# Scoring the second router during the last expert of the first layer

## The chip, the cores and the metric

The program runs on one core of a Trainium2 chip. Its engines are named as in the profile: PE is TensorE (matrix products and, against an identity, transposes), PEld its weight load, ACT is ScalarE, DVE is VectorE, POOL is GpSimd, SP is SyncE, which here only issues transfers. The metric is the time of one execution on the device, in microseconds (us); lower is better.

## The reference

Three blocks follow each other on 1536 tokens of 512 numbers, in fp32. Block 1 is an attention with a window and four sink positions. Blocks 2 and 3 are mixtures of 8 experts (two matrices of 512 x 1024 and 1024 x 512 each). What matters here is the end of block 2 and the start of block 3:

```python
# block 2, in _moe_ref: two experts for each token
for e in range(E):
    for k in range(2):
        mask = top2[:, k] == e
        h = np.maximum(x[mask] @ w1[e], 0.0)
        out[mask] += top2_w[mask, k, None] * (h @ w2[e])
# block 3, in _moe2_ref, on x = out of block 2: one expert for each token
logits = x @ w_gate + modality_bias[modality_id]
e_idx = np.argmax(logits, axis=1)
gate_w = softmax(logits)[np.arange(N), e_idx]
```

Block 3's choice needs the complete sum over all experts of block 2, but its scores are linear in that sum.

## The kernel before

**First layer (block 2).** Each expert e owns 416 places ("slots"), in four groups of rows (k = 0 to 3; three of 128 and one of 32). `first1(e, f)` makes one of 8 pieces of the hidden layer, transposed, with 12 products of 416 columns. `second1(e, d)` makes one of 4 pieces of the expert's output with 24. Numbers are split into a high and a low part (fp32r), and so three products stand for one: ACT copies the high part out of PSUM (`relu1`, `x1_high_part`), DVE computes the low part (`h1_low_part`, `x1_low_part`). ACT copies each finished piece into `yT` (`y1_copy`). `back(e, k)` transposes `yT` into rows of tokens, `y_scale(e, k)` multiplies them by the gate on DVE into one of two row buffers, and `scatter1(e, k)` on POOL adds the rows to `x_moe1` in HBM with an indirect transfer. This way back of expert e-1 is interleaved with `first1(e, f)`, at f = 0, 2, 4, 6. `y_scale` waits until the scatter two places earlier has landed, since it writes the same buffer.

**Overflow.** Tokens that find no slot are treated by `over_layer`, which reads a count at run time and branches over its whole body when that is zero; with these inputs it is zero. PE, ACT, DVE and POOL each have such a branch, and SP one too. Before the change those of PE, ACT, DVE and POOL stand after expert 7.

**Between the layers.** When all scatters have landed, POOL raises `all_scattered`. SP then loads the 12 tiles of 128 tokens back (`x2_loads`, into `x2_rows`), PE transposes them (L1121), ACT and DVE split them (L1554, L2147), `group_scores` (L1104) multiplies by the second router's weights in three groups of four tiles, `turned_scores` (L1112) turns the scores to rows of tokens, and DVE adds the bias (`biased_scores`, L2143). `keep_clock_up(30)` (L770) is filler on PE for the time in which it waits for the tiles.

**Routing (after that).** `pick` (from L1765) finds each token's expert, `place_tokens(1)` its place, POOL writes one table (`coded_tiles`, L551) and DVE another (L1842), PE multiplies them (`codes2`, L881), and POOL gathers the rows of the first tile (L646). SP loads the first expert's weights once `order` is known. The second layer then runs over tiles.

Each engine runs its own program in order and is held only by semaphores, so the order in the code is that of the work.

## Time and profile before

| | us |
|---|---|
| three runs, median | 691.99 (690.84 to 693.63) |
| profiled execution, its own time | 693.64 |
| span of the profiled execution | 691.90 |
| PE busy, all of the span | 647.2 |
| expert 7, from its first product to its last | 414.91 to 452.91 |
| from there to the start of `pick` | 452.91 to 488.64 |
| first product of the second layer | 505.64 |

The span is what the trace covers. The execution's own time is 1.74 us more than it. Starts in the trace are counted from the span's start.

### The profile page before, as it was taken

How to read it: one execution, taken by the hardware profiler on the slowest of the kernel's cores; microseconds unless marked ns; L12 is line 12 of the kernel's file. 1: busy time of each engine (PE TensorE's matmuls, PEld its weight loads, DVE VectorE, ACT ScalarE, POOL GpSimd, SP SyncE). 2: the span in 40 equal slices, each digit the busy share in tenths (PEclk: the TensorE clock that was granted, in tenths of full speed). 3: DMA queues.
4: the chain of work that ended last, by engine and by line, in shares of the span. 5: the costliest groups of instructions: out<-in, count | busy, mean ns of one | idle time of the engine just before them, and what ended most of it. 6: DMA issues, size and time to landing. Idle time of an engine off the chain costs nothing. (4 is left out here: it accounts for less than half of the span.)

```text
span 691.9 us, 11241 instructions
## 1 busy us (share of the span) xinstructions
PE 647.2 (94%) x3822; PEld 581.3 (84%) x3823; DVE 317.1 (46%) x642; ACT 273.5 (40%) x525; POOL 183.1 (26%) x194
## 2 busy tenths in 40 slices
PE   8989999998999999999999999967489999999994
PEld 6989998897999999999999999944268888788883
DVE  4566646585456436262543624114684422452221
ACT  5768766333434244352524333104155321441210
POOL 2500100137172615425161512030131221221201
PEclk9999999999999999999999999999799999999998
DMA  7777630454584645556564502035396410001100
GB/s 212 266 271 259 222 118 23 169 170 133 172 245 153 146 139 113 180 153 185 152 155 123 108 3 34 12 47 182 122 358 221 157 56 31 30 24 42 46 15 26
DMA packets 52095, 91.21 MB, mean 132 GB/s; under 512 B 8591, under 2 KB 14735, under 8 KB 52048
## 3 DMA queue, kind: packets, MB, share of 16 engines
q1 hardware_dynamic: 41872, 69.21, 29.8%
q0 software_dynamic: 10176, 21.38, 13.9%
q8 instruction: 29, 0.48, 0.3%
q14 instruction: 18, 0.15, 0.1%
HBM read 74.52 MB, written 18.40 MB: 134 GB/s over the span
## 5 line engine op out<-in xcount | busy, mean ns | idle before, releaser
L588 POOL DMA_INDIRECT x_moe<-rows,dst_idx x29 | 57.8, 1994 | 138.0 <-DVE rows L1977 135.9
L1588 DVE TENSOR_TENSOR split<-stage,split 128x2048 fp32r<-128x2048 f32 x32 | 73.3, 2290 | 41.8 <-ACT split L1255 41.7
L900 PE MATMUL banks<-xTs,split 128*128 128x416 f32 (+1 forms) x256 | 88.6, 350 | 0.8 <-issue 0.8
L901 PE MATMUL banks<-xTs,split 128*128 128x416 f32 (+1 forms) x256 | 86.4, 342 | 0.0
L958 PE MATMUL banks<-hTs,split 128*128 128x416 f32 x224 | 79.6, 355 | 0.0
L959 PE MATMUL banks<-hTs,split 128*128 128x416 f32 x224 | 78.5, 351 | 0.0
L1390 ACT ACTIVATE hTs<-banks 128x416 fp32r<-128x416 f32 x56 | 29.0, 518 | 82.6 <-PE banks L903 82.6
L1255 ACT ACTIVATE split<-stage 128x2048 fp32r<-128x2048 f32 x32 | 60.9, 1908 | 0.5 <-DMA stage<-w1a 0.5
L1477 ACT ACTIVATE hTs<-banks 128x512 fp32r<-128x512 f32 x28 | 16.6, 597 | 108.0 <-PE banks L1178 108.0
L903 PE MATMUL banks<-xTs,split 128*128 128x416 f32 (+1 forms) x256 | 56.2, 340 | 0.0
L705 PE MATMUL banks<-k_sb,q_sb 128*128 128x260 f32 (+2 forms) x192 | 49.9, 386 | 2.9 <-DMA k_sb<-k_w 1.5
L1598 DVE CUSTOM_DVE_ANT_0 negs<-banks,masks 128x260 f32<-128x260 f32 (+2 forms) x96 | 35.0, 402 | 35.9 <-PE banks L705 34.6
L1750 DVE SCALAR_TENSOR_TENSOR hTs<-banks,hTs 128x416 fp32r<-128x416 f32 x56 | 32.8, 587 | 36.3 <-ACT hTs L1390 36.2
L900 PEld LDWEIGHTS banks<-xTs,split 128*128 128x128 f32 x256 | 48.1, 188 | 1.3 <-issue 1.0
L662 POOL DMA_INDIRECT out<-rows,dst x14 | 14.3, 1020 | 131.5 <-DVE rows L2070 131.5
L1268 ACT ACTIVATE probs<-negs,negmax 128x260 f32<-128x260 f32 (+2 forms) x96 | 46.1, 484 | 7.3 <-DVE negmax L1598 7.1
L901 PEld LDWEIGHTS banks<-xTs,split 128*128 128x128 f32 x256 | 48.2, 188 | 0.3
L1950 DVE TENSOR_TENSOR xTs<-banks,xTs 128x512 fp32r<-128x512 f32 (+1 forms) x28 | 16.6, 592 | 68.0 <-ACT xTs L1359 45.0
L965 PE MATMUL banks<-hTs,split 128*128 128x416 f32 x224 | 47.7, 355 | 0.0
L1163 PE MATMUL banks<-split,xTs 128*128 x112 | 45.3, 405 | 2.3 <-DVE split L1584 1.6
L903 PEld LDWEIGHTS banks<-xTs,split 128*128 128x128 f32 x256 | 46.2, 187 | 0.3
L1189 PE MATMUL banks<-split,hTs 128*128 x112 | 45.0, 402 | 0.6 <-ACT hTs L1477 0.6
(292 smaller groups left out, 1290.2 us busy)
## 6 DMA issues: line engine op xcount, KB each, us to landing
stage<-w1a SPq DMA_DIRECT2D x16, 1024.0 KB
stage<-w2a SPq DMA_DIRECT2D x16, 1024.0 KB, 5.5
k_sb<-k_w SPq DMA_DIRECT2D x12, 520.0 KB, 4.5
raw<-w1b SPq DMA_DIRECT2D x6, 1024.0 KB
raw<-w2b SPq DMA_DIRECT2D x6, 1024.0 KB, 7.0
q_sb<-q_t SPq DMA_DIRECT2D x24, 128.0 KB, 3.5
x_attention<-rows SPq DMA_DIRECT2D x12, 256.0 KB, 5.5
split<-x_moe SPq DMA_DIRECT2D x12, 256.0 KB, 5.2
```

Of the source, the lines that this page charges most:

```text
L588: pool.indirect_dma_start(out=x_dram[1], out_offset=rows_at(dst_idx[0], early_dst, e, k), in_=y_room(n), in_offset=None, compute_op=ALU.ad ...
L705: mm = pe.matmul(S[:, j % 2, h, 0:n], q_sb[:, b, pair, h, :], k_sb[:, b, pair, 0:n], start=True, stop=True)
L900: pe.matmul(psum, piece(slot, 0, o + c * FH), xTs[:, 0, c, 0:cols], start=(c == 0), stop=False)
L901: pe.matmul(psum, piece(slot, 1, o + c * FH), xTs[:, 0, c, 0:cols], start=False, stop=False)
L903: mm = pe.matmul(psum, piece(slot, 0, o + c * FH), xTs[:, 1, c, 0:cols], start=False, stop=(c == DC - 1))
L958: pe.matmul(psum, piece(e % 2, 0, o), hTs[:, 0, c, 0:cols], start=(c == 0), stop=False)
L959: pe.matmul(psum, piece(e % 2, 1, o), hTs[:, 0, c, 0:cols], start=False, stop=False)
L965: mm = pe.matmul(psum, piece(e % 2, 0, DC * F + c * D + d * P), hTs[:, 1, c, 0:cols], start=False, stop=(c == FC - 1))
L1163: pe.matmul(psH[:, half, :], xTs2[:, 0, c, :], weights(slot, 0, o), start=(c == 0), stop=False)
L1255: act.activation(split_chunk(e % 2, 0, c), staged_chunk(e % 2, c), ACT.Copy).then_inc(high_done[c], 1)
L1268: act.activation(probs[:, b, 2 * pair + h, 0:span(kind)], negs[:, j % 2, h, 0:span(kind)], ACT.Exp, bias=negmax[:, j % 2, h:h + 1], scale= ...
L1588: dve.tensor_tensor(split_chunk(e % 2, 1, c), staged_chunk(e % 2, c), split_chunk(e % 2, 0, c).bitcast(F32), ALU.subtract).then_inc(low_do ...
```

## The change

The second router's scores are computed in two parts. The rows that lack only expert 7's share are loaded, transposed and scored while PE works on expert 7. Expert 7's share comes another way: `last_logits(d)` multiplies its unscaled outputs in `yT` by the router's weights in fp32, giving 8 scores for each slot; DVE multiplies these by the gate and cuts them in three bf16 parts (`last_tokens`); `last_to_tokens` adds them to their tokens with 48 products against one-hot tables that DVE makes of the slots' tokens (`last_away`, `last_one_hot`); DVE sums everything. What goes with it:

- `most_scattered` is raised when the scatters up to expert 6 have landed, and `x2_loads` waits for that. Its buffer is now a ring of 8 tiles in expert 6's weight room; tiles 8 to 11 wait for a transpose each.
- The way back of expert 6 stands at f = 0, 1, 2, 3 of expert 7.
- All `over_layer` parts now stand between expert 6 and expert 7 (on POOL ahead of expert 6's scatters).
- Expert 7's rows are turned into four banks and scaled by ACT (`last_scale`), no longer by DVE. Its scatters stay ahead of `coded_tiles(1)` on POOL.
- `keep_clock_up(30)` goes.

```diff
-        x2_rows = split[:, 1, 0].bitcast(F32)[:, 0:TILES * D].rearrange("p (t d) -> p t d", d=D)
+        x2_ring = split[:, 0, :, DC * TILES * P:].bitcast(F32).rearrange("p k (t d) -> p k t d", d=D)
@@ SP
-            sp.wait_ge(all_scattered, 1)
+            sp.wait_ge(most_scattered, 1)
             for t in range(TILES):
+                if t >= 8:
+                    sp.wait_ge(x2t, t - 7)
+                sp.dma_start(x2_row(t), x_dram[1][t * P:(t + 1) * P, :]).then_inc(x2_in[t % 8], 16)
@@ POOL
             for e in range(1, E):
+                if e == E - 1:
+                    over_layer()
                 for k in range(SUBS if e > 1 else EARLY_SUBS + 1):
                     scatter1(e - 1, k)
+                if e == E - 1:
+                    all_landed(nth_sub(e, 0))
+                    pool.sem_inc(most_scattered, 1)
@@ PE, new functions
+            def x2_transposes(t):
+                pe.wait_ge(x2_in[t % 8], 16 * (t // 8 + 1))
+                if t >= 4:
+                    pe.wait_ge(x2t_low, t - 3)
+                for c in range(DC):
+                    mm = pe.transpose(ps2T[:, t % 4, c * P:(c + 1) * P], x2_row(t)[:, c * P:(c + 1) * P], ident[:])
+                mm.then_inc(x2t, 1)
+            def last_logits(d):
+                pe.wait_ge(y1_copied, DC * (E - 1) + d + 1)
+                if d == 0:
+                    pe.wait_ge(scaled1, nth_sub(E - 1, 0))
+                for k in range(SUBS):
+                    first = min(k * P, SLOTS - P)
+                    mm = pe.matmul(psLast[:, k, :], yT[:, d, first:first + P], wg2[:, d, :], start=(d == 0 and k == 0),
+                                   stop=(d == DC - 1 and k == SUBS - 1), skip_group_check=True)
+            def last_to_tokens():
+                pe.wait_ge(last_hots, SUBS)
+                pe.wait_ge(last_parted, 1)
+                for t in range(TILES):
+                    for k in range(SUBS):
+                        mm = pe.matmul(psMore[:, t, :], last_hot[:, k, t, :], last_parts[:, k].rearrange("p n e -> p (n e)"),
+                                       start=(t == 0 and k == 0), stop=(t == TILES - 1 and k == SUBS - 1), skip_group_check=True)
+                mm.then_inc(last_added, 1)
@@ PE, the experts
+                    elif e == E - 1 and f < SUBS:
+                        pe.wait_ge(scaled1, nth_sub(e - 1, f))
+                        back(e - 1, f, psO1)
...
+                if e == E - 2:
+                    over_layer()
+            last = E - 1
+            second1(last, 0)
+            for t in range(3):
+                x2_transposes(t)
+            second1(last, 1)
+            last_logits(0)
+            for t in range(3, 7):
+                x2_transposes(t)
+            second1(last, 2, groups=(0,))
+            last_logits(1)
+            for t in range(7, TILES):
+                x2_transposes(t)
+            second1(last, 3, groups=(1, 2))
+            last_logits(2)
+            turned_scores()
+            last_logits(3)
             for k in range(SUBS):
-                pe.wait_ge(scaled1, nth_sub(E - 1, k) - (k > 0))
-                back(E - 1, k, (psO1, psX1)[k % 2])
+                back(last, k, banks[:, k + 1, :])
+            last_to_tokens()
-            keep_clock_up(REST_LAYER, psH1[:, 0, :])
@@ ACT, expert 7 (x2_high is the copy that stood in L1554, turned_copy that of L1550)
+                y1_copy(last, 0)
+                for t in range(3):
+                    x2_high(t)
+                y1_copy(last, 1)
...
+                y1_copy(last, 3)
+                for k in range(SUBS):
+                    last_scale(k)
@@ DVE, after expert 7's low parts (x2_low is the operation of L2147)
+                last_away()
+                for t in range(TILES):
+                    x2_low(t)
+                    if t % 3 == 2:
+                        last_one_hot(t // 3)
+            def last_tokens():
+                dve.wait_ge(last_lg_ready, 1)
...
+                link(dve.tensor_tensor(last_parts[:, :, 2, :], last_rest, last_parts[:, :, 1, :], ALU.subtract))
+                dve.sem_inc(last_parted, 1)
+                dve.wait_ge(lg2, 1)
+                link(dve.tensor_tensor(noisy[:], ps2, bias_tok[:], ALU.add))
+                dve.wait_ge(last_added, 1)
+                link(dve.tensor_reduce(rb[:], psMore.rearrange("p t (n e) -> p t e n", e=E), AX.X, ALU.add))
+                link(dve.tensor_tensor(noisy[:], noisy[:], rb[:], ALU.add))
```

On PE's program, the place between expert 6's last products (L965 before, L992 now) and expert 7's first (L900 and L901 before, L925 and L926 now). Before:

```order
L965 MATMUL banks<-hTs,split 128x416 x8
L900 MATMUL banks<-xTs,split 128x416
L901 MATMUL banks<-xTs,split 128x416
```

Of the change, first the branch and then, behind the body that it jumps over, the end of the body and the products that follow:

```order
L992 MATMUL banks<-hTs,split 128x416 x8
L1095 TENSOR_LOAD used
L1095 ISA x2
L1096 COMPARE_AND_BRANCH
...
L1096 UNCONDITIONAL_BRANCH
L925 MATMUL banks<-xTs,split 128x416
L926 MATMUL banks<-xTs,split 128x416
```

The load of the count and the branch over the overflow's body now stand between two products that followed each other directly.

On PE's program, from expert 7's last products to the first product of the routing (L860 before, L885 now). Before:

```order
L965 MATMUL banks<-hTs,split 128x416 x8
L1018 MATMUL banks<-ident,yT 128x128 x16
L1069 TENSOR_LOAD used
L1069 ISA x2
L1070 COMPARE_AND_BRANCH
...
L770 MATMUL banks<-ones_bf 128x512 x30
L1121 MATMUL banks<-ident,split 128x128 x24
L1104 MATMUL banks<-split,wg_parts 16x512 x8
L1121 MATMUL banks<-ident,split 128x128 x16
L1104 MATMUL banks<-split,wg_parts 16x512 x8
...
L860 MATMUL banks<-chosen,ones_bf 128x8 x12
```

And of the change:

```order
L992 MATMUL banks<-hTs,split 128x416 x8
L1027 MATMUL banks<-wg,yT 128x8 x4
L1018 MATMUL banks<-both,rows 128x8 x12
L1027 MATMUL banks<-wg,yT 128x8 x4
L1091 MATMUL banks<-ident,yT 128x128 x16
L1037 MATMUL banks<-chosen,last_hot 128x24 x48
L885 MATMUL banks<-chosen,ones_bf 128x8 x12
```

The transposes of the token tiles and their scores are gone from this stretch; four sets of fp32 products come, two of them here (L1027), and the 48 one-hot products (L1037; the parts are kept in `chosen`).

On POOL's program, from the overflow's count to the first table of the routing, with the semaphores that each waits for. Before, expert 6's and expert 7's scatters, the count, the table:

```order
L588 DMA x_moe<-rows,dst_idx 1664x512 [waits scaled1,scattered1_1,scattered1_0]
L588 DMA x_moe<-rows,dst_idx 1664x512 [waits scaled1] x3
L621 TENSOR_LOAD used [waits fresh_ready0,scattered1_1,scattered1_0]
...
L551 TENSOR_TENSOR moving<-xT,code 128x12x19 [waits hot_ready]
```

And of the change:

```order
L613 TENSOR_LOAD used [waits fresh_ready0]
...
L603 DMA x_moe<-rows,dst_idx 1664x512 [waits scaled1,scattered1_1,scattered1_0]
L603 DMA x_moe<-rows,dst_idx 1664x512 [waits scaled1] x3
L603 DMA x_moe<-rows,dst_idx 1664x512 [waits scattered1_0,scattered1_1,scaled1]
L603 DMA x_moe<-rows,dst_idx 1664x512 [waits scaled1] x3
L567 TENSOR_TENSOR moving<-xT,code 128x12x19 [waits scattered1_0,scattered1_1,hot_ready]
```

The count moved ahead of both experts' scatters; the table still waits until expert 7's scatters have landed.

## Rows read from the trace of the kernel before

**Rows 1.** The page, busy time of each engine over the span.

```profile
PE 647.2 (94%) x3822; PEld 581.3 (84%) x3823; DVE 317.1 (46%) x642; ACT 273.5 (40%) x525; POOL 183.1 (26%) x194
```

**Rows 2.** Busy time by stretch: length, engines, granted clock (1.00 is full), DMA share, GB/s.

```profile
414.91:452.91 38.00, 38.00 (x209) 37.20 (x208) 9.80 (x14) 7.94 (x13) 6.33 (x4) 1.00 0.16 21
452.91:488.64 35.73, 25.80 (x142) 14.96 (x142) 11.31 (x19) 8.72 (x16) 6.27 (x4) 0.95 0.43 111
488.64:505.64 17.00, 7.06 (x58) 3.52 (x59) 13.41 (x45) 5.08 (x5) 3.71 (x7) 0.70 0.55 182
461.00:463.00 2.00, 2.00 (x6) 0.64 (x5) 0.00 (x0) 0.00 (x0) 1.69 (x2) 0.50 1.02 138
463.00:465.00 2.00, 2.00 (x9) 0.85 (x8) 0.00 (x0) 0.00 (x0) 0.15 (x1) 0.81 0.62 92
```

**Rows 3.** The chain that ended last, in order of time: start, length, what.

```profile
461.59 4.65 DMA x_moe<-rows,dst_idx
...
467.60 0.34 SPq L361
...
486.50 1.89 PE banks L1112 x16
...
488.64 0.27 DVE top L1765
```

**Rows 4.** The timeline of PE: start, length, what, count, idle before.

```profile
451.24 1.67 PE L965 MATMUL banks<-hTs,split 128*128 128x416 f32 x8
455.08 1.32 PE L1018 MATMUL banks<-ident,yT 128*128 128x128 f32 x8 [0.41 <-DVE rows L1977]
460.85 8.06 PE L770 MATMUL banks<-ones_bf 128*128 128x512 bf16 x30 [4.46 <-issue]
470.35 0.66 PE L1121 MATMUL banks<-ident,split 128*128 128x128 f32 x4 [1.44 <-DMA split<-x_moe]
477.41 1.91 PE L1121 MATMUL banks<-ident,split 128*128 128x128 f32 x16
480.02 2.01 PE L1104 MATMUL banks<-split,wg_parts 128*16 128x512 f32 x8 [0.70 <-DVE split L2147]
```

**Rows 5.** Two branches on PE's queue, by line: durations in ns, starts.

```profile
L1070 PEldq COMPARE_BRANCH  x1: 4037/4037/4037, 456.8 to 456.8; - x1
L1233 PEldq COMPARE_BRANCH  x5: 77/208/208, 623.4 to 673.6; - x5
```

**Rows 6.** Queue of instruction transfers (packets, MB, share), in 416:417 and in 458:459.

```profile
q8 instruction: 1, 0.02, 8.2%
q8 instruction: 1, 0.02, 5.9%
```

**Rows 7.** The timeline, small products on PE and a sum on DVE.

```profile
59.80 1.02 PE L764 MATMUL banks<-wg,xT 128*128 128x16 f32 x8
498.00 0.56 PE L881 MATMUL banks<-moving,row_hot 128*128 128x38 bf16 x12 [6.77 <-DVEq L1849]
498.74 0.31 DVE L1783 TENSOR_REDUCE owner_f<-shared 128x19 f32<-128x152 f32 x1
```

**Rows 8.** The timeline, expert 7: ACT behind `first1(7, 1)` and `(7, 2)`, POOL's first scatter.

```profile
420.04 0.52 ACT L1390 ACTIVATE hTs<-banks 128x416 fp32r<-128x416 f32 x1 [2.17 <-PE banks L903]
422.29 0.52 ACT L1390 ACTIVATE hTs<-banks 128x416 fp32r<-128x416 f32 x1 [1.74 <-PE banks L903]
424.98 0.52 ACT L1390 ACTIVATE hTs<-banks 128x416 fp32r<-128x416 f32 x1 [2.17 <-PE banks L903]
421.80 1.62 POOL L588 DMA_INDIRECT x_moe<-rows,dst_idx  x1 [20.21 <-DVE rows L1977]
```

**Rows 9.** The timeline, the two tables of the second routing.

```profile
495.71 0.57 POOL L551 TENSOR_TENSOR moving<-xT,code 128x228 bf16<-128x228 f32 x1 [32.56 <-DVEq L1839]
495.71 2.18 DVE L1842 TENSOR_TENSOR row_hot<-row_i,iota_row 128x1536 bf16<-128x1536 int32 x1
```

**Rows 10.** Transfers to and from `x_moe`, issue to landing.

```profile
DMA to landing us min/median/max: 2.7/4.9/12.2
```

More of the change, by code:

```diff
@@ L584, in scatter1 @@
                 if k == 0 and e > 0:
[L585 to L586 removed]
+                    all_landed(n)
                 pool.wait_ge(scaled1, n + 1)
@@ L944, in early_second_low, with second1 @@
                 mm.then_inc(y1, 1)
-            def second1(e, d, between=None):
+            def second1(e, d, between=None, groups=()):
                 cols = SLOTS
@@ L961, in second1 @@
                     x1_transposes(e + 1, between)
+                for g in groups:
+                    group_scores(g)
                 for c in range(FC):
@@ L966, in second1, with group_scores @@
                 mm.then_inc(y1, 1)
+            def x2_transposes(t):
[5 more added lines that the diff above has]
+                mm.then_inc(x2t, 1)
+            def group_scores(g):
+                pe.wait_ge(x2t_low, (g + 1) * GROUP)
+                if g == 1:
+                    pe.wait_ge(lg2t_copied, g)
+                for c in range(DC):
+                    for k in range(2):
+                        mm = pe.matmul(ps2L[g], wg2_parts[:, c].rearrange("p k e -> p (k e)"),
+                                       x2T[:, k, c, g * GROUP:(g + 1) * GROUP, :].rearrange("p t n -> p (t n)"),
+                                       start=(c == 0 and k == 0), stop=(c == DC - 1 and k == 1))
+                mm.then_inc(lg2t, 1)
@@ L1055, in _ @@
                             back(0, k, psO1)
-                    elif f % 2 == 0:
+                    elif e < E - 1 and f % 2 == 0:
                         pe.wait_ge(scaled1, nth_sub(e - 1, f // 2))
                         back(e - 1, f // 2, psO1)
-                for d in range(DC):
-                    more = e < E - 1
-                    second1(e, d, {1: 1, 2: 3}.get(d) if more else None)
-                    if more and d < 2:
-                        x1_transposes(e + 1, 2 * d)
-            for k in range(SUBS):
-                pe.wait_ge(scaled1, nth_sub(E - 1, k) - (k > 0))
-                back(E - 1, k, (psO1, psX1)[k % 2])
@@ new lines, in first_layer @@
+                    if more:
+                        for d in range(DC):
+                            if d in (1, 2):
+                                x1_high_part(e + 1, 2 * d - 1)
+                            y1_copy(e, d)
+                            if d < 2:
+                                x1_high_part(e + 1, 2 * d)
+                            else:
+                                first_layer_high(e + 1, d)
+                    if e == E - 2:
+                        over_layer()
+                last = E - 1
@@ new lines, in first_layer @@
+                y1_copy(last, 0)
+                for t in range(3):
+                    x2_high(t)
+                y1_copy(last, 1)
+                for t in range(3, 7):
+                    x2_high(t)
+                turned_copy(0)
+                y1_copy(last, 2)
+                for t in range(7, TILES):
+                    x2_high(t)
+                turned_copy(1)
+                turned_copy(2)
+                y1_copy(last, 3)
+                for k in range(SUBS):
+                    last_scale(k)
```

327 lines of the change are left out of this document (168 added, 159 removed).

## The prediction

> **What bounds the kernel now.** I first read the page's engine shares: PE is busy 94% of the span and all others are below half [rows 1], so a change is worth what it takes off PE's idle or wasted time, or off a chain on which PE waits. Then the busy times by stretch. In expert 7 PE is busy 38.00 of 38.00 us at full clock, with DVE, ACT and the transfers nearly free. In the 35.73 us between expert 7's last product and `pick` it is busy 25.80, and 8.06 of these are the 30 filler products [rows 2, 4]. The routing behind that is a chain on DVE, 17.00 us long, which the change leaves as it is [rows 2]. Third, the chain that ended last, between 453 and 489: the last scatter lands at 461.59 + 4.65 = 466.24, SP issues the loads from 467.60, PE starts on the tiles at 470.35, and the last turned scores end at 488.39 [rows 3, 4]. So this stretch waits on a round trip through HBM, and then on PE, ACT and DVE in turn; the filler costs nothing there. The change puts the round trip and the tiles' work under expert 7, where PE has no idle time: what PE does in there lengthens it in full.
>
> **The change part by part.** I count PE's time from 452.91, the end of expert 7's last product, to `pick`; 35.73 us before. A product that follows its like is priced by the start-to-start time of its row.
>
> What stays or comes, on PE, all of it uncovered:
> - Twelve tiles of four transposes: 16 took 1.91 us, so 0.48 for a tile, 5.7 us [rows 4].
> - Three groups of scores of 8 products: 2.01 us each, 6.0 us [rows 4].
> - Twelve turned scores: 16 took 1.89 us, so 1.4 us [rows 3].
> - Sixteen fp32 products of `last_logits` with 8 columns. No row has these; the nearest is the first router's, fp32 with 128 x 128 weights and 16 columns, 8 in 1.02 us, so 2.0 us. The 0.118 us of a turned score as a lower end gives 1.9.
> - Four ways back: a `first1` with one takes 424.98 - 422.29 = 2.69 us and one without 422.29 - 420.04 = 2.25, so 0.44 each, 1.8 us [rows 8].
> - 48 one-hot products in bf16, 24 columns. The nearest is `codes2`, bf16, 38 columns, 12 in 0.56 us, so 2.2 us; at the price of the fp32 row it would be 6.1, the upper end [rows 7]. I take the bf16 row.
> - DVE's end: a sum over 288 numbers (0.31 us for 152 [rows 7], so some 0.45), an addition like the 0.27 us steps of `pick` [rows 3], and about 0.2 for two semaphores: 0.95 us. DVE's five small steps on the slots' scores, some 1.3 us, lie under the four ways back (1.8); without that cover they would cost 1.3.
>
> Together 20.05 us.
>
> What is moved: the overflow's branch. On PE the gap around it is 456.40 to 460.85, 4.45 us, 4.04 of it the branch instruction itself [rows 4, 5]. Before, that lay in the time in which PE waited for the tiles anyway. Now it stands between two products that followed each other without a gap, and nothing hides it: +4.45. Other branches of PE take 0.08 to 0.21 us [rows 5]. They jump over one tile's step; this one jumps over about 200 matrix products with their weight loads. A transfer of instructions stands in the microsecond from 458 on, inside the long branch [rows 6]: I read it as the code behind the body being fetched. The body is as long as before. In the undisturbed stream a transfer also stands in 416:417, some 1.5 us behind the branch's new place [rows 6], so the code there is near the end of what was brought in, and the target is again beyond what follows. The Trainium skill, "Advanced Engine Details and Errata" (Control Flow Timing), gives about 108 ns for a compare-and-branch. By that price the gap would be about 0.5 us and the sum 4 us smaller. The Trainium skill, "Runtime: NRT & Kernel Launch" (Instruction fetch mechanics), says that a taken branch whose target is outside the fetched window stalls until it is brought in. By that the 4.45 comes again; the trace agrees with it, with 4.04 us against 0.21.
>
> The clock: after the gap at 456.40 the granted clock is 0.50 in 461 to 463 and 0.81 in 463 to 465 [rows 2], that is at 1.2 GHz until about 463.76, or 2.9 us after work resumed, half of which is lost: +1.45 us for the same gap ahead of expert 7. Ahead of it PE is busier than it was ahead of 456.40, so the fall may not come; the bounds are 0 and 1.45, and I take 1.45, as the only gap of this length had it.
>
> ACT, DVE and POOL have their own branches in the same place. They wait for PE there and have short bodies; I cost them at nothing, and DVE's low parts have until four `first1` later.
>
> Waits that come in. `y_scale(6, 2)` needs the first scatter's buffer. That scatter started at 421.80 [rows 8] and landed 4.65 us on [rows 3], at 426.45, and its scale takes some 0.7. PE, with a way back behind each `first1`, wants that scale for `back(6, 3)` at 424.98 + 0.44 = 425.4 [rows 8], so it would wait 1.8 us. But the gap on PE gives DVE time to catch up, so that the first scatter can start closer behind PE; then nothing is left of the wait. I take 0.3 and keep 0 and 1.8 for the range. Behind the waiting scale on DVE stands the low part of f = 3, needed only by `first1(7, 7)`. With the shift of 5.9 us and the late start kept, the first scatter starts at 427.7, the second 2.69 later at 430.4, and lands at 435.05; the fourth waits for that and starts some 1.6 later, landing at 441.3. SP issues the loads 0.4 on, and the first tile is there 2.75 us after its issue (470.35 against 467.60 [rows 3, 4]), near 444.5. PE wants it after `second1(7, 0)`: 414.91 [rows 2] plus 8 x 2.25, 4 x 0.44, 4.56 for the 24 products (a quarter of what is left of the 38.00) and 6.2 of gap, clock and wait, so 445.4. Hidden, with 0.9 us to spare. The last tiles wait a little on DVE's pace: 0.2. Together +0.5.
>
> On POOL the first table waits for expert 7's scatters. The first scale starts about 4.6 us ahead of `pick`, the fourth scatter is issued near 2.6 us after it and lands near 7.3. The table was made 495.71 - 488.64 = 7.07 after `pick` and takes 0.57, and PE needs it only with DVE's table, which ends 2.18 us after it starts [rows 9]. So 7.9 against 9.3: hidden by 1.4 us. The gather is later still, and so the whole rest moves with `pick`.
>
> The sum: 20.05 + 4.45 + 1.45 + 0.5 = 26.45 us against 35.73, that is -9.3 us. The profiled execution's span of 691.90 becomes 682.6 and its time of 693.64 becomes 684.3. The median of the runs lies 1.65 below that execution, so I forecast 691.99 - 9.3 = 682.7. A measurement of this kernel can tell about 0.5%, or 3.5 us, from no change.
>
> **The rivals.**
>
> (a) *The forecast*, 682.7, with 681 to 687 for the open prices: the clock that may not fall (-1.45), the wait of `back(6, 3)` (up to +1.5), one-hot products at up to 6.1 (+3.9, of which I allow 3). Chance 0.63.
>
> (b) *The moved branch is cheap.* If the target's code is at hand in the new place, the branch costs the 0.21 us of PE's others, and the clock doesn't fall: 682.7 - 3.8 - 1.45 = 677.4. For it: all other branches. Against it: the same body, and rows 6. By the 108 ns of the Trainium skill, "Advanced Engine Details and Errata" (Control Flow Timing), this would be the case. Chance 0.15.
>
> (c) *POOL becomes the bound after `pick`.* If a scatter of expert 7 takes not 4.65 us but the longest landing of `x_moe`, 12.2 us [rows 10], the table is 7.5 later, less the 1.4 spare: 682.7 + 6.1 = 688.8, the same as before or just faster. The long landing may be one of the large transfers to `x_moe`, and in this stretch little else moves until the weights' loads. Chance 0.09, with all cases in which half or more of the gain is lost to some wait.
>
> (d) *Slower: the scatters of expert 6 hold PE.* They go in two rounds, each waiting for the one before. Each us that a landing takes beyond 4.65 brings the tiles 2 us later, less the 0.9 spare, and PE stands in expert 7 waiting for the first tile. At 12.2 us: 2 x 7.55 - 0.9 = 14.2, so 696.9. The gain is gone from a landing of about 9.8 us on, and the kernel slower by 0.5% from 11.5. Against it: the transfers are busy 0.16 in expert 7 [rows 2], and 4.65 was measured with four scatters in a row. Chance 0.06.
>
> (e) *The change does little*, since the fp32 products or the table of expert 7 take several times their nearest rows: 687 to 690. Chance 0.07.
>
> **How the numbers follow.** The likeliest is (a), 682.7. From 676.5, below (b), to 688, short of (c), lie (a), (b) and about half of (e): 0.8. Faster by over 0.5% is below 688.5: (a), (b), and half of (c) and (e), 0.86. Within 0.5%: 0.08. Slower: (d), 0.06.
>
> **What the profile after would show.** A gap of about 4.4 us on PE between L992 and L925 and a long branch at L1096, with a granted clock of 0.5 for some 3 us behind it (right for (a)); none of the two (b). PE without a wait for tiles at L1000 (d would show it there, and on DVE a long wait ahead of the scale of group 2). Expert 7, gap aside, about 15 us longer. From the end of the last L992 product to `pick` some 7.5 us where it was 35.73. `L567` no later than about 8 us after `pick`'s start and L906 no later than 9.4 (c shows otherwise). I would be wrong above all if the one-hot products or `last_logits` are far from their rows, or the landing is slower with the new rhythm.

## The result, and the profile after

Times in us, each median over the runs of the same session on one chip, with the ratio of the changed kernel to the kernel before and its 95% interval:

| session | before | changed | ratio |
|---|---|---|---|
| first | 692.62 (690.84 to 693.63) | 684.15 (682.01 to 686.54) | 0.9881 [0.9832, 0.9931] |
| second | 692.0 | 683.17 (682.49 to 689.22) | 0.9892 [0.986, 0.9925] |
| third | 691.62 | 683.87 (681.05 to 686.87) | 0.989 [0.9864, 0.9917] |

The change saves 7.8 to 8.8 us, 1.1 to 1.2%. The profiled execution took 682.12 us, with a span of 680.2. It lies 2.0 below its median, where that of before lay 1.0 above the median in the table (1.65 above that of the three runs known ahead of the prediction), so the difference of the two spans, 11.7 us, is larger than what the change gives. What follows is therefore read by stretches. Most of the spread between runs lies ahead of the place that was changed: in the thirteen profiles of the changed kernel and its variants, whose code is the same up to there, expert 6's last product ends between 412.4 and 417.5, while from there to `pick` the three profiles of the changed kernel took 62.90, 62.73 and 62.91 us. What sets the time ahead of it is open.

The page of the changed kernel, busy time of each engine and the granted clock in 40 slices. PE has 50 more instructions and is busy 1.6 us less than in [rows 1]:

```profile
PE 645.6 (95%) x3872; PEld 585.2 (86%) x3873; DVE 322.6 (47%) x651; ACT 276.2 (41%) x529; POOL 185.5 (27%) x194
PEclk9999999999999999999999999998599999999997
```

Busy time by stretch of the changed kernel (columns as in [rows 2]): expert 7; from its last product to `pick`; from `pick` to the second layer's first product; and four pieces of the second stretch:

```profile
414.50:466.36 51.86, 51.03 (x299) 46.74 (x299) 24.19 (x33) 14.84 (x27) 6.33 (x4) 1.00 0.30 77
466.36:476.20 9.84, 8.96 (x105) 8.75 (x103) 1.91 (x8) 3.27 (x5) 2.70 (x2) 0.83 0.11 13
476.20:493.89 17.69, 8.37 (x58) 3.92 (x59) 13.58 (x45) 5.19 (x5) 9.26 (x10) 0.61 0.84 227
470.00:471.00 1.00, 1.00 (x10) 1.00 (x11) 0.05 (x1) 0.00 (x0) 0.00 (x0) 1.00 0.00 0
471.00:472.00 1.00, 1.00 (x8) 1.00 (x7) 0.86 (x5) 0.43 (x1) 0.00 (x0) 0.57 0.00 0
472.00:474.00 2.00, 2.00 (x13) 1.94 (x12) 0.28 (x2) 1.63 (x3) 0.81 (x1) 0.50 0.00 0
474.00:475.00 1.00, 1.00 (x43) 1.00 (x42) 0.00 (x0) 0.69 (x1) 0.77 (x1) 0.72 0.00 0
```

Against [rows 2], expert 7 is 13.86 us longer (51.86 for 38.00), the way to `pick` 25.89 shorter (9.84 for 35.73), and the routing 0.69 longer. The routing's end is a gather that landed after 3.91 us in this run. What follows it, to the end of the span, is 186.31 us long, and was 186.26. So the gain lies in the place that was predicted; of the 11.7 us between the spans 1.8 are none of it, since expert 6's last product already ended at 413.30 for 415.07. The last four lines show what was not: PE is busy without a break, and the granted clock falls from full to half at about 471.1.

The timeline of PE in the changed kernel (start, length, what, count, idle before), from expert 6's last products to the codes. L1091 is a way back, L1000 the tiles' transposes, L1009 the group scores, L1027 `last_logits`, L1018 the turned scores, L1037 the one-hot products, L906 `codes2`:

```profile
411.63 1.67 PE L992 MATMUL banks<-hTs,split 128*128 128x416 f32 x8
414.50 0.43 PE L925 MATMUL banks<-xTs,split 128*128 128x416 f32 x1 [1.21 <-issue]
...
425.70 0.66 PE L1091 MATMUL banks<-ident,yT 128*128 128x128 f32 x4 [0.63 <-DVE rows L2067]
...
439.77 1.47 PE L1000 MATMUL banks<-ident,split 128*128 128x128 f32 x12
...
464.69 1.67 PE L992 MATMUL banks<-hTs,split 128*128 128x416 f32 x8
466.20 0.95 PE L1027 MATMUL banks<-wg,yT 128*128 128x8 f32 x8
467.08 2.84 PE L1018 MATMUL banks<-both,rows 16*128 16x8 f32 x24
469.86 1.06 PE L1027 MATMUL banks<-wg,yT 128*128 128x8 f32 x8
470.77 3.32 PE L1091 MATMUL banks<-ident,yT 128*128 128x128 f32 x16
473.88 1.43 PE L1037 MATMUL banks<-chosen,last_hot 128*128 128x24 bf16 x48
...
485.83 0.56 PE L906 MATMUL banks<-moving,row_hot 128*128 128x38 bf16 x12 [6.57 <-DVEq L1940]
```

The reader is to see three things. PE stands idle 1.21 us where the branch is now, not 4.45. The first tile's transposes (L1000) wait for nothing. And the counts of L1027 and L1018 are twice those of the code: four fp32 products of `last_logits(d)` are 8 records, 12 turned scores are 24.

By line, the branch and the load of its count on PE's own queue in the changed kernel (durations in ns, starts); the like of before is in [rows 5]:

```profile
L1096 PEldq COMPARE_BRANCH  x1: 3712/3712/3712, 410.6 to 410.6; - x1
L1095 PEldq TENSOR_LOAD <-used x1: 488/488/488, 409.8 to 409.8; - x1
```

The branch is nearly as long as it was, 3.71 us for 4.04. But it starts at 410.6, while the last product of expert 6 ends at 411.63 + 1.67 = 413.30: PE's queue had come to it 2.7 us before the array had worked off the products ahead of it, and only what outlasts them is seen.

### The profile page after: what moved, and what is told of

It is laid out like the page before. It is cut to its first block, busy times and chain, and to the rows that moved or that the text cites. A ratio compares the mean times of both kernels' runs of the same rounds, so it can differ in the third digit from the quotient of the medians.

```text
span 680.2 us, 11358 instructions
## 1 busy us (share of the span) xinstructions
PE 645.6 (95%) x3872; PEld 585.2 (86%) x3873; DVE 322.6 (47%) x651; ACT 276.2 (41%) x529; POOL 185.5 (27%) x194
## 4 chain that ended last, share of the span: by engine, by line
PE 83%; DVE 6%; DMA 3%; ACT 2%; issue 2%; SPq 1%; ACTq 0%; POOL 0%; DVEq 0%; POOLq 0%
PE banks L984 6%; PE banks L983 6%; PE banks L992 6%; PE banks L925 5%; PE banks L926 5%; PE banks L928 5%; PE banks L730 5%; PE banks L758 4%; PE banks L1234 4%; PE banks L1239 4%; PE banks L1235 4%; PE banks L1260 4%; PE banks L1261 4%; PE banks L1264 3%; PE banks L742 2%
## 5 line engine op out<-in xcount | busy, mean ns | idle before, releaser
L925 PE MATMUL banks<-xTs,split 128*128 128x416 f32 (+1 forms) x256 | 88.9, 352 | 2.0 <-issue 2.0
L926 PE MATMUL banks<-xTs,split 128*128 128x416 f32 (+1 forms) x256 | 86.4, 342 | 0.0
L925 PEld LDWEIGHTS banks<-xTs,split 128*128 128x128 f32 x256 | 48.1, 188 | 2.9 <-issue 2.5
L926 PEld LDWEIGHTS banks<-xTs,split 128*128 128x128 f32 x256 | 48.2, 188 | 0.3
L992 PE MATMUL banks<-hTs,split 128*128 128x416 f32 x224 | 47.7, 355 | 0.0
L2191 DVE TENSOR_TENSOR hTs<-banks,hTs 128x512 fp32r<-128x512 f32 x28 | 19.2, 690 | 58.0 <-ACT hTs L1581 57.1
```

The lines of the kernel that those rows point to most:

```text
L925: pe.matmul(psum, piece(slot, 0, o + c * FH), xTs[:, 0, c, 0:cols], start=(c == 0), stop=False)
L926: pe.matmul(psum, piece(slot, 1, o + c * FH), xTs[:, 0, c, 0:cols], start=False, stop=False)
L992: mm = pe.matmul(psum, piece(e % 2, 0, DC * F + c * D + d * P), hTs[:, 1, c, 0:cols], start=False, stop=(c == FC - 1))
```

## The experiments

Each was run beside the kernel before on the same chip; a ratio is always to that. The first four were run in the second session of the table, the next four in one with a median before of 694.18 and without the changed kernel (so only their ratios are compared), the last four in the third of the table. "First product to `pick`" is the time from expert 7's first product to the start of `pick`, in the profiled execution. It is 61.70 us in the changed kernel, and was 73.73.

**The changed kernel again**, as the base of the next three experiments and for the spread.

> The changed kernel itself, for its spread: its four runs were 682.0, 682.1, 686.2 and 686.5 us, with mean granted clocks of 0.983, 0.982, 0.977 and 0.978. Theory: the 4 us between the two groups are one more stretch at half clock (0.0055 of 684 us is 3.8 us of full clock lost), so each run here falls in one of the two groups and its time follows its clock. Rival: the groups differ at equal clock, by transfers.

683.17, ratio 0.9892. First product to `pick` 61.92, the idle time at the branch 0.81, the wait of the fourth way back 1.22. So single profiles of one kernel differ by half a microsecond in these waits, while their sum stays (1.84 and 2.03, and 1.89 in the third profile below). The times fall in no two groups by their clock: three runs with a mean granted clock of 0.981 took 682.70, 683.48 and 685.76.

**Without PE's branch.** It leaves out PE's part of the overflow (with these inputs it has nothing to do).

```diff
             for e in range(1, E):
 ...
-                if e == E - 2:
-                    over_layer()
```

> Leaves out PE's part of the overflow layer, its branch included (unused with these inputs). Theory: the branch hides behind the products that PE has queued, and costs the 1.2 us that the trace after shows as a gap ahead of expert 7's first product, so 1.2 us are saved. Rival, as the prediction had it: the branch costs 4.45 us and 1.45 of clock, so up to 5.9 us are saved.

682.27, ratio 0.9858 [0.9834, 0.9882]: by the medians 0.9 us faster than the changed kernel beside it, and within its spread. The gap is gone, and two waits for DVE's scales stand in its place:

```profile
414.75 0.60 PE L1091 MATMUL banks<-ident,yT 128*128 128x128 f32 x4
418.56 0.66 PE L1091 MATMUL banks<-ident,yT 128*128 128x128 f32 x4 [0.96 <-DVE rows L2065]
421.34 0.60 PE L1091 MATMUL banks<-ident,yT 128*128 128x128 f32 x4
425.04 0.66 PE L1091 MATMUL banks<-ident,yT 128*128 128x128 f32 x4 [0.83 <-DVE rows L2065]
```

The pause at the branch had given DVE time, as the prediction supposed; without it PE waits 1.79 us for the scales, and 1.22 for one of them in the kernel above. From expert 6's last product to `pick` it is 62.80 us, for 62.73 to 62.91 with the branch: the 1.2 us expected are not saved there, let alone 5.9.

**The branch without its head start.** One wait holds PE's queue ahead of the branch until ACT has copied expert 6's last piece, so that nothing is queued behind which the branch could run.

```diff
                 if e == E - 2:
+                    pe.wait_ge(y1_copied, DC * (E - 1))
                     over_layer()
```

> PE waits until expert 6's last piece has been copied, and only then comes to the branch; nothing is queued behind which it could hide. Theory (the head start is what makes the branch cheap): the gap becomes some 5 us (0.7 for the copy, 0.7 for the count, 3.7 for the branch) against 1.2, +3.9 us, and the granted clock may fall behind it, +1.5 more; 688 to 690. Rival (the branch is cheap in its new place for another reason, such as code that is at hand): +0.7 us for the wait alone.

688.13, ratio 0.9949 [0.993, 0.9967]: 4.96 us slower than the changed kernel beside it, as the head start would have it. In its timeline and its windows:

```profile
412.41 1.67 PE L992 MATMUL banks<-hTs,split 128*128 128x416 f32 x8
419.42 0.69 PE L925 MATMUL banks<-xTs,split 128*128 128x416 f32 x1 [5.34 <-issue]
```

```profile
414.08:419.42 5.34, 0.01 (x1) 0.04 (x1) 2.45 (x2) 2.31 (x2) 0.00 (x0) 0.72 0.02 3
419.42:422.42 3.00, 3.00 (x9) 2.87 (x10) 0.00 (x0) 0.00 (x0) 0.00 (x0) 0.50 0.02 5
```

The same branch (3.69 us here) costs a gap of 5.34, and behind it 3 us at half clock, which are the two terms of the prediction (4.45 and 1.45) come true. What the prediction lacked is the head start, and this one edit takes it away. Some 0.6 us of the gap are the edit's own, since it also waits for ACT's copy (the load of the count starts at 414.7, the products end at 414.08).

**One-hot products between the ways back.** Expert 7's second pair of ways back goes behind `last_to_tokens`, so that DVE's end lies beside it.

```diff
-            for k in range(SUBS):
+            for k in range(2):
                 back(last, k, banks[:, k + 1, :])
             last_to_tokens()
+            for k in range(2, SUBS):
+                back(last, k, banks[:, k + 1, :])
```

> Two of expert 7's four ways back stand behind the 48 one-hot products instead of ahead of them. Theory (PE's order up to pick is the bound there): pick starts 1.6 us earlier after expert 7's last product, as two ways back took 1.6 us at half clock. On POOL the fourth scatter is issued no later, since POOL takes 1.87 us for each, but its landing now holds the first table: 1.2 to 1.6 us saved. Rival (POOL's wait for the scatters is already the bound): nothing saved, since the first table cannot come earlier than the landing.

684.01, ratio 0.9867 [0.9842, 0.9893], the same as the changed kernel; the 1.2 to 1.6 us expected do not show. `pick` comes no sooner in this run (first product to `pick` 62.39), since the clock fell 2.6 us behind expert 7's last product, in the turned scores already, ahead of the first thing that the edit moves. And the codes now wait for POOL, at the time at which they came anyway (9.79 us after `pick`, for 9.45 to 9.98 in the three profiles of the changed kernel):

```profile
PE banks L906 <- POOL moving L567: 7.1, 1, 7.1
```

The table came 8.32 us after `pick` (7.34 in the changed kernel), since the scatters ahead of it started later relative to `pick`. It cost nothing here; the account of POOL's table below says why.

**Turned scores earlier.** Two thirds of the turned scores go between the group scores and the last eight products of expert 7, to have fewer small products in a row behind it.

```diff
+                if len(groups) > 1:
+                    turned_scores((0, 1))
...
-            turned_scores()
+            turned_scores((2,))
```

> The turned scores of the first two groups stand inside expert 7's last piece, among its wide products, and only the third group's behind it. PE's work is the same. Theory (the granted clock falls in the tail because PE runs only small products for about 4.8 us there): with 2.9 us of them left ahead of the ways back, the clock stays at 1.00 until the ways back, which take 1.8 us and not 2.8 to 3.2, and from the last product of expert 7's piece to pick it is 9.8 - 1.85 - 1.2 = 6.7 us; the whole from expert 7's first product to pick is 1 to 1.5 us shorter. Rival (the clock falls at its own times): the whole is the same as before, 61.7 to 62 us.

686.03, ratio 0.9892 [0.9861, 0.9924]. The clock fell all the same, 3.4 us behind the last product, and the ways back took 2.98 us. So fewer small products in a row did not keep it up in this run. First product to `pick` is 63.12, longer than either theory had it, and 2.06 of it are a wait of the fourth way back of expert 6 for its scale, ahead of everything that the edit moves.

**Both of these.**

> The early turned scores together with two ways back behind the one-hot products. Theory: the tail is shorter by the 1.2 of the clock and by 0.9 for two ways back at full clock; but the first table waits for the fourth scatter's landing, which is 1.2 to 1.6 us later relative to pick, so part of it comes back as a wait of codes for POOL: 1 to 2 us below the changed kernel, 681 to 682. Rival (POOL holds it all): no more than the early turned scores alone.

685.17, ratio 0.9861 [0.9831, 0.989], not to be told from the changed kernel. First product to `pick` 61.62. In this run the clock stayed full until after the first pair of ways back (1.07 us for two, 1.95 for the two at half clock), and yet next to nothing was won up to `pick` (61.61 to 61.92 in the changed kernel); why is open. The codes waited for POOL's table again (6.6 us), but came 9.49 us after `pick`, no later than in the changed kernel.

**Expert 6's ways back at the old, even places.** This puts them behind `first1` 0, 2, 4, 6 as before, so that each scale finds its buffer free, but the scatters come later.

```diff
-                    elif e < E - 1 and f % 2 == 0:
+                    elif f % 2 == 0:
...
-                    elif e == E - 1 and f < SUBS:
-                        pe.wait_ge(scaled1, nth_sub(e - 1, f))
-                        back(e - 1, f, psO1)
```

> Expert 6's way back stands at f = 0, 2, 4, 6 of expert 7 again, everything else as changed. Theory: the wait of 0.6 to 1.2 us of PE for the third scale goes, but the fourth scatter is issued about 5.5 us later (434.5), lands at 439.2, and the first tile is there at 442.3 where PE wants it at 439.9 less the wait: 2 to 3 us of waiting for tiles appear, net 1 to 2 us slower. Rival (the landing has slack enough): 0.6 to 1.2 us faster.

689.36, ratio 0.9943 [0.9922, 0.9964]. First product to `pick` 67.03, which is 5.3 more, where 1 to 2 were expected. Counted from expert 7's first product (418.49 in this run, 414.50 in the changed kernel), the fourth scatter starts after 19.95 us for 14.10, SP's loads after 23.74 for 18.03, and PE waits for the first tile. The timeline of PE and two windows:

```profile
444.99 2.20 PE L1000 MATMUL banks<-ident,split 128*128 128x128 f32 x12 [1.93 <-DMA split<-x_moe]
```

```profile
446.00:448.00 2.00, 1.89 (x10) 1.62 (x9) 1.43 (x3) 1.48 (x3) 0.00 (x0) 0.69 0.90 306
448.00:450.00 2.00, 2.00 (x7) 1.89 (x7) 2.00 (x2) 0.00 (x0) 0.00 (x0) 0.50 1.03 370
```

A wait of 1.93 us is followed by some 3 us at half clock, which costs about 1.5 us more. That is rival (d)'s place, reached by a later start instead of a slower landing. It shows that a tile's wait would have been dear. Not all of the 5.3 us is the price of the rhythm, though: 1.9 lie behind expert 7's last product (11.76 us to `pick` for 9.84), where the clock fell 3.7 us behind it for 4.8.

**Filler among the turned scores.** Ten filler products of 512 columns, two behind every second score.

```diff
                 for t in range(TILES):
 ...
+                    if t < TILES - 1 and t % 2 == 1:
+                        keep_clock_up(2, banks[:, 1, :])
```

> Ten filler products of 512 columns (2.1 us) stand between the turned scores. Theory (it is the small products that let the clock fall): the granted clock stays 1.00 through the ways back, which then take 1.8 us and the one-hot products less too; from expert 7's end to pick 9.8 + 2.1 - 1.5, so about 10.5 us: 0.6 slower, with the clock up. Rival (the clock falls at its own times): the clock falls all the same, and the tail is 2.1 us or more longer.

689.9, ratio 0.9939 [0.99, 0.9978]. The clock fell at about 471.0, in the middle of the filler, and stayed low:

```profile
469.00:471.00 2.00, 2.00 (x12) 1.19 (x12) 0.00 (x0) 0.00 (x0) 0.00 (x0) 0.98 0.00 0
471.00:473.00 2.00, 2.00 (x7) 1.05 (x6) 0.00 (x0) 0.00 (x0) 0.00 (x0) 0.50 0.00 0
```

From expert 7's last product to `pick` it took 16.56 us for 9.84. The ten fillers themselves took 3.6 us, start to start, for the 2.1 expected, and the small products and ways back behind them more than before, at half clock. Filler on the critical path cost three times its price and bought nothing.

**The changed kernel a third time**, as the base of the last three.

> The changed kernel once more, as the base of the three others on this chip. Every theory expects a ratio to the kernel before of about 0.989 (0.986 to 0.993), expert 7's first product to pick 61.7 to 62.0 us.

683.87, ratio 0.989, first product to `pick` 61.61.

**Four rooms for expert 6's rows.** Groups 2 and 3 are scaled into `x_rows`, free at that time, and need not wait for the first scatters (POOL's scatters read them there).

```diff
...
+                own = e == E - 2 and k >= 2
-                if n >= 2:
+                if n >= 2 and not own:
...
-                dve.tensor_scalar(y_rows[:, n % 2], rows_in,
+                dve.tensor_scalar(x_rows[:, k - 2] if own else y_rows[:, n % 2], rows_in,
```

> Expert 6's third and fourth group of rows are scaled into a room of their own, so that DVE's scales of these groups no longer wait until the scatters of the first two have landed. Theory (the wait ahead of back(6, 3) is the only idle time of PE in expert 7 that the change brought): the idle time of 0.6 us (0.35 to 2.1 in the runs so far) ahead of the last way back of expert 6 is gone, the tiles' loads are issued earlier by 1 to 4 us, and the stretch from expert 7's first product to pick is 0.6 to 1.5 us shorter than in the changed kernel on this chip, ratio to the kernel before some 0.001 to 0.002 lower. Rival: the idle time is replaced by another (the way back waits on DVE's pace in any case, or the clock falls as much later), and the stretch stays within 0.3 us.

682.94, ratio 0.9867 [0.9841, 0.9893]. PE's waits of expert 7 in the changed kernel, and then in this one (line waited for: us in total, times, longest):

```profile
PE banks L925 <- issue: 1.2, 1, 1.2
PE banks L1091 <- DVE rows L2067: 0.6, 1, 0.6
PE banks L1000 <- DVE split L2109: 0.2, 1, 0.2
```

```profile
PE banks L927 <- issue: 0.8, 1, 0.8
PE banks L1002 <- DVE split L2112: 0.2, 1, 0.2
```

The wait is gone, and expert 7 takes 51.15 us for 51.85 in the changed kernel beside it. But in this run the clock fell 3.8 us behind the last product instead of 4.9, and the way to `pick` took 10.80 for 9.76. So expert 7's gain is shown in the trace; in the whole time, 0.9 us between medians is less than the spread.

**No share at all.**

```diff
-            last_logits(0)
...
-            last_to_tokens()
```

(and DVE's steps on them, and its sum).

> Leaves out expert 7's share of the scores altogether: no fp32 products of its slots, no one-hot products, none of DVE's steps on them, no sum; the second router then chooses from scores without that share, so places and tables can differ. It prices the way by which the share comes. Theory (all of it is uncovered on PE): 3.3 us of fp32 products, 1.24 of one-hot products, 0.75 of DVE's end go, so pick comes 5 to 6 us sooner behind expert 7's first product, and the kernel is 4 to 6 us faster than the changed one if POOL's table holds. Rival 1: pick no longer waits for the ways back, so it comes sooner still (by 3 more us, 8 to 9), but POOL's table, which waits for the scatters behind these ways back, then holds the codes' products; the gain up to the codes is then only 2 to 4 us. Rival 2: part of the share's way lies beside other work, and the gain is under 3 us throughout.

680.86 (680.70 to 681.19), ratio 0.9838 [0.9808, 0.9868], 3.0 us faster by the medians, though the two intervals just meet. First product to `pick` is 54.32, 7.3 us less; but the codes come 16.74 us after `pick` for 9.98, so that expert 7's first product to the codes is 71.06 for 71.59. The chain of this kernel, in order of time, shows what took over:

```profile
470.53 1.36 POOL x_moe L603
...
476.15 8.19 DMA x_moe<-rows,dst_idx
484.54 0.58 POOL moving L567
485.21 0.55 PE banks L906 x12
```

Rival 1 holds: of 7.3 us, 0.5 are left at the codes in this pair of profiles (and 1.2 at the second layer's first product, 77.84 for 79.04), less than the 2 to 4 that it named. The medians differ by its 3.0; the profile of the changed kernel beside it was the lowest of its six runs, so how much is left in the others is open. The last of its four scatters landed only after 8.19 us here, and the table waits for it. What came in its way can be read: with `pick` earlier, SP issued the second layer's first two weight loads of 1 MB each at 476.56, 0.41 us behind this scatter, and the transfers moved 316 GB/s from 480 to 484. In the three profiles of the changed kernel the loads came 2.8 to 3.7 us behind the last scatter. That they made it slow is likely, but no run held them back. The share's way on PE and DVE, and the scatters on POOL, run side by side and are nearly equal in length, so taking one away is worth little. That is rival (c), half a step away.

**Four rooms and the split together.**

> The four rooms together with expert 7's one-hot products moved between its second and third way back (their DVE end then lies beside two ways back). If both small gains hold and add, the ratio to the kernel before is about 0.985 to 0.987, that is 1.5 to 3 us faster than the changed kernel on this chip; from expert 7's last product to pick some 1.5 us less. Rival: POOL's table then comes as the last (8.3 us after pick or later, since the scatters start later relative to pick), and the gain of the split is lost to it: the ratio is that of the four rooms alone.

681.12 (680.07 to 685.26), ratio 0.9841 [0.9816, 0.9866]. The changed kernel beside it had 0.989 [0.9864, 0.9917]: five of its six runs lie below 683.0, and only one of the changed kernel's six does. The means are 681.9 and 684.0. The profiled run was its slowest, 685.26, and has the split's known end:

```profile
483.54 1.15 POOL L567 TENSOR_TENSOR moving<-xT,code 128x228 bf16<-128x228 f32 x1 [2.72 <-POOLq L663]
...
492.56 1.09 PE L1219 MATMUL banks<-ident,rows 128*128 128x128 f32 x4 [3.17 <-DMA rows<-x_moe,src]
```

First product to `pick` is 61.05, 0.6 less. The table starts 8.55 us after `pick`, the codes come after 9.79 as without the split, and the transposes ahead of the second layer's first product waited 3.17 us for their rows, for 0.71 and 1.60 in the first two profiles of the changed kernel. So by its median this is the best version of those that compute everything, 2.75 us below the changed kernel, and likely but not surely better; each half alone could not be told from the changed kernel.

## Why the prediction was right, and where its terms were not

The forecast was 682.7, 9.3 us below; measured were 7.8 to 8.8 below, with 684.15 well inside the range. Rival (a) holds as a picture: the round trip and the tiles' work are hidden under expert 7, `pick` comes close behind it, and the rest moves with `pick`. From the end of expert 6's last product to `pick`, the changed kernel took 476.20 - 413.30 = 62.90 us against 488.64 - 415.07 = 73.57: 10.7 us less in these two profiles, where the sum said 9.3. With 0.4 to 0.7 us lost in the routing, some 10 us are left at the second layer's first product, in all three profiles of the changed kernel; the medians say 7.8 to 8.8. There is one profile of before, and what the rest is stays open. The terms, in us:

| term | predicted | measured |
|---|---|---|
| branch | 4.45 | 1.2 (0.8 to 1.3 in three profiles) |
| clock behind it | 1.45 | 0 |
| twelve tiles | 5.7 | 5.3 |
| three group scores | 6.0 | 5.55 |
| `last_logits` | 2.0 | 3.4 |
| turned scores | 1.4 | 2.8 |
| ways back of expert 7 | 1.8 | 3.1 |
| one-hot products | 2.2 | 1.4 |
| DVE's end | 0.95 | 0.8 |
| waits in expert 7 | 0.5 | 0.8 |

These add to 24.35 us; the stretch itself is 25.06 (62.90 less the 37.84 from expert 6's end to expert 7's before), so 0.7 is not placed. The sum of the prediction was 26.45. The result is near the forecast because two groups of errors nearly cancel: 4.7 us too much for the branch and its clock, 4.1 too little for the small fp32 products and the ways back. The place of the gain was foreseen; that the total comes so near is luck.

**The moved branch (mis-sized, 4.45 + 1.45 against 1.2 + 0).** The step said that the branch "now stands between two products that followed each other without a gap, and nothing hides it". The products queued ahead of it hide it: its start, 410.6, is 2.7 us ahead of the end of expert 6's last product. The run that took the head start away had a gap of 5.34, half clock for 3 us behind it, and lost 4.96 us. In [rows 4, 5] it had no such cover. The last ways back, which end at 455.08 + 1.32 = 456.40, had waited for DVE's scale (0.41 us), so little was queued, and the branch started at 456.8, behind their end. So rival (b) was near with the size of the gap and wrong about its reason: the branch is not cheap, 3.3 to 3.8 us in four profiles of the new place, it is covered. Why it takes so long wasn't tried; that code is fetched, as [rows 6] was read, stays a reading. For it: in all five profiles read for this (before, the changed kernel three times, and the run without a head start) a transfer of instructions starts 0.6 to 1.7 us behind the branch's start, 411.5 to 412.0 in the changed kernel, and the run without PE's branch has none there. The price of the Trainium skill, "Advanced Engine Details and Errata" (Control Flow Timing), about 108 ns, fits neither place; by it, the gap of 5.34 could not be there. The Trainium skill, "Runtime: NRT & Kernel Launch" (Instruction fetch mechanics), describes a stall for a target that isn't at hand; the trace agrees in kind, with 3.3 to 4.0 us and the transfer inside them, but the page names no length.

**Small fp32 products (mis-sized).** `last_logits` is 0.80 to 0.91 us for four products, 0.21 each, and a turned score 0.23, where I took 0.125 and 0.118. The counts in the rows misled me: an fp32 product with moving columns leaves two records, so the row of the first router, x8 in 1.02 us [rows 7], is four products, and the x16 of [rows 3] eight turned scores, not sixteen. The code would have told: `x_logits` makes 4 products in each of 12 blocks, and the trace of before has 96 records of that line. Read so, the same rows give 16 x 0.255 = 4.1 us, an upper bound for half as many columns (3.4 measured), and 12 x 0.236 = 2.8 (2.8). The transposes leave one record each, which is why the ways back and tiles did not suffer from this.

**The ways back of expert 7 (mis-sized, by the clock).** Their 1.8 us became 3.1 since the granted clock was at half from 471.1, with PE busy in all of the time before. The prediction put the low clock behind the branch; it came behind the small products instead. In all thirteen profiles, of six different orders of this end, it fell between 2.6 and 5.4 us after expert 7's last product, and neither fewer small products nor ten wide fillers among them prevented it. Nine of the thirteen have the same work on PE from that product to the fall, and these nine alone span the whole range. So the order of the end is not what sets the moment, and one profile of an order cannot show that it moved it; what does set it is open.

**One-hot products** took 1.4 us, partly at half clock: 30 ns each, below the bf16 row. The upper end of 6.1 was far off.

**Waits.** The wait of the fourth way back is there, 0.6 us (0.59 to 1.22 in the three profiles of the changed kernel), within its bounds of 0 and 1.8; in the run with the turned scores earlier it was 2.06. The first tile had more to spare than predicted: issue at 432.53, wanted at 439.77, so some 4.5 us for 0.9. The forecast had kept the late start of before (421.80 [rows 8], 6.9 us behind expert 7's first product) and added 5.9 us of gap and clock. The first scatter started at 420.06, 5.6 us behind, and nearly all of the 5.9 was not there. SP's loads followed the fourth scatter's start by 3.93 us, too, where the forecast had 4.65 + 0.4. Rival (d) was therefore further off than it looked, and the run with even places shows what it would have cost.

Rival (e) had a grain of truth: the fp32 products cost 1.7 and 2 times what I took, which is 2.8 us, short of the 4 or more that it wanted.

**POOL's table** was done 7.91 us after `pick`, for 7.9 predicted (its start was at 7.34), and the codes waited for DVE (L1940), as said. But the forecast took the two tables as independent, and they are not. In the changed kernel's first and second profile:

```profile
483.54 2.18 DVE L1933 TENSOR_TENSOR row_hot<-row_i,iota_row 128x1536 bf16<-128x1536 int32 x1
483.54 0.57 POOL L567 TENSOR_TENSOR moving<-xT,code 128x228 bf16<-128x228 f32 x1 [3.16 <-DVEq L1930]
...
483.93 1.76 DVE L1933 TENSOR_TENSOR row_hot<-row_i,iota_row 128x1536 bf16<-128x1536 int32 x1
484.00 2.13 POOL L567 TENSOR_TENSOR moving<-xT,code 128x228 bf16<-128x228 f32 x1 [2.67 <-POOLq L661]
```

Started together, POOL's table takes 0.57 us and DVE's 2.18. Started 0.07 us later, POOL's takes 2.13 and ends 0.44 behind DVE's, which takes 1.76. In the two splits and in the run with both edits POOL's starts 0.36 to 1.05 later and again ends 0.43 or 0.44 behind. So they take turns (what makes them was not tried), and any lateness makes POOL's the last, in the changed kernel itself too. It costs nothing up to 1.05 us: the codes start 2.29 us behind DVE's table in all five of these profiles. Only without the share, where POOL's table started 6.5 us late, did it hold the codes.

## What to carry to other kernels

A branch, or any long instruction of an engine's queue, costs only what outlasts the work already queued ahead of it: look for its start in the queue's rows, and compare it with the end of that work, ahead of pricing a move. Where a stall is taken away, look for the next releaser of the same instruction within a microsecond: here the branch, DVE's scales and POOL's scatters each stood ready to take over, and removing one gave back little of its length (at the codes, 0.5 us of 7.3 in the profiles without the share). Where an engine is named as the one that was waited for, look also whether the work came later than before: POOL was named in four profiles in which nothing was lost. And ahead of pricing by a row's count, check what one record is against a loop whose count the code tells.

## What the runs showed of the hardware

- The granted clock fell from 2.4 to 1.2 GHz although PE was busy 100% of each microsecond, among fp32 products with 8 columns and transposes, 2.6 to 5.4 us behind the last product of 416, and over all of this range in nine profiles with the same work; and it fell with ten products of 512 columns among the small ones too.
- A taken branch on PE over a body of some 200 matrix products with their weight loads took 3.3 to 4.0 us in five profiles, in either place. With products queued ahead, PE stood idle for 0.8 to 1.3 us of it; with none, 5.34, of which 0.6 are that run's own.
- An indirect scatter landed after 4.74 us as the first of four (changed kernel), after 4.65 [rows 3] and 8.19 us as the fourth of four (before, and without the share; in the latter two loads of 1 MB were issued 0.41 us behind it).
- Two table operations on DVE and POOL took turns: 2.18 and 0.57 us when started together, 1.76 and 1.15 to 2.13 when POOL's started 0.07 to 1.05 us later.
